# Attention tiles and feed-forward slices on one core: a longer tile pipeline, half weight loads, later stores, slices spread over all steps

## What is computed

```python
scores = scale * q @ k.T
kth = np.partition(scores, -32)[..., -32]
scores = np.where(scores >= kth, scores, -1e9)
x = softmax(scores) @ v
h = x @ w_in; x = (h * sigmoid(h)) @ w_out
P = exp(logits - max); 8 rounds of row and column scaling
out = sum over 8 experts of P[:, e] * (relu(x @ w1[e]) @ w2[e])
```

## Time and profile before

| what | value |
|---|---|
| median of three runs | 1378.49 us |
| the profiled execution | 1377.77 us |
| its span | 1376.0 us |
| mean granted TensorE clock | 0.968 |
| TensorE busy | 93% |
| VectorE busy | 50% |
| ScalarE, POOL busy | 30%, 27% |

### The profile page before, as it was taken

How to read it: one execution, slowest core, us unless ns; L and a number is a source line. 1 busy time by engine, 2 the same in 40 slices (tenths; PEclk the granted TensorE clock), 3 DMA queues, 4 the chain that set the end, 5 groups by cost and what they waited for, 6 DMA issues and landing times.

```text
span 1376.0 us, 21031 instructions
## 1 busy us (share of the span) xinstructions
PE 1284.8 (93%) x8029; PEld 1133.4 (82%) x8029; DVE 691.8 (50%) x1557; ACT 416.3 (30%) x888; POOL 365.4 (27%) x317
## 2 busy tenths in 40 slices
PE   5766699979979999999999999999999999999999
PEld 4555588768758889989989989989988988988997
DVE  6876899989999952652222222222222222222222
ACT  3433455445545523302202202202211211210210
POOL 2544433343434423202202202202202211211200
PEclk9987799989989999999999999999999999999999
DMA  4655514562543636211001001101101101101001
GB/s 122 210 201 188 197 71 172 192 210 88 229 158 138 246 129 245 73 51 61 32 31 62 30 30 61 42 19 61 61 0 61 61 0 61 61 22 39 0 0 69
DMA packets 72288, 130.12 MB, mean 95 GB/s; under 512 B 41376, under 2 KB 41376, under 8 KB 63008
## 3 DMA queue, kind: packets, MB, share of 16 engines
q1 hardware_dynamic: 72224, 129.27, 26.7%
HBM read 110.12 MB, written 19.14 MB: 94 GB/s over the span
## 4 chain that ended last, share of the span: by engine, by line
PE 75%; DVE 12%; POOL 6%; issue 3%; ACT 2%; DMA 2%; SPq 0%; ACTq 0%; DVEq 0%
PE banks L396 23%; PE banks L397 22%; PE banks L398 22%; DVE stats L838 5%; DVE rest L849 4%; PE banks L440 2%; POOL probs L1088 2%; DMA wu_raw<-in_moe_w_in_dram 2%; PE banks L464 1%; POOL wu_lo L1068 1%; PE banks L431 1%; DVE probs L860 1%; PE banks L549 1%; POOL wd_lo L1068 1%; POOL xt_lo L1094 1%
## 5 line engine op out<-in xcount | busy, mean ns | idle before, releaser
L798 ACT ACTIVATE h_hi<-banks 128x384 fp32r<-128x384 f32 x192 | 94.4, 492 | 624.6 <-PE banks L398 624.6
L396 PE MATMUL banks<-x_lo,wu_hi 128*128 128x384 f32 x768 | 257.2, 335 | 0.0
L398 PE MATMUL banks<-x_hi,wu_hi 128*128 128x384 f32 x768 | 256.8, 334 | 0.0
L397 PE MATMUL banks<-x_hi,wu_lo 128*128 128x384 f32 x768 | 256.8, 334 | 0.0
L1068 POOL TENSOR_TENSOR wu_lo<-wu_raw,wu_hi 128x512 fp32r<-128x512 f32 x76 | 95.9, 1300 | 580.7 <-ACT wu_hi L741 573.8
L969 DVE SCALAR_TENSOR_TENSOR h_lo<-banks,h_hi 128x384 fp32r<-128x384 f32 x192 | 106.8, 557 | 281.4 <-ACT h_hi L798 281.4
L1011 DVE SCALAR_TENSOR_TENSOR y_acc<-banks,plan_e,y_acc 128x512 f32<-128x512 f32 x135 | 101.4, 751 | 272.3 <-PE banks L398 272.3
L396 PE MATMUL banks<-wd_lo,h_hi 128*128 128x512 f32 x576 | 227.9, 396 | 0.0
L398 PE MATMUL banks<-wd_hi,h_hi 128*128 128x512 f32 x576 | 227.8, 396 | 0.0
L397 PE MATMUL banks<-wd_hi,h_lo 128*128 128x512 f32 x576 | 227.8, 396 | 0.0
L838 DVE MAX8 stats<-rest 128x8 f32<-128x576 f32 x216 | 156.1, 750 | 0.1
(11 more groups left out here) (102 smaller groups left out, 1876.3 us busy)
## 6 DMA issues: line engine op xcount, KB each, us to landing
wu_raw<-in_moe_w_dram SPq DMA_DIRECT2D x16, 1024.0 KB, 5.0
wd_raw<-in_moe_w_dram SPq DMA_DIRECT2D x16, 1024.0 KB, 5.1
wu_hi<-kept_up_hi SPq DMA_DIRECT2D x14, 1024.0 KB, 5.6
wu_lo<-kept_up_lo SPq DMA_DIRECT2D x14, 1024.0 KB, 7.8
wd_hi<-kept_down_hi SPq DMA_DIRECT2D x14, 1024.0 KB, 5.6
wd_lo<-kept_down_lo SPq DMA_DIRECT2D x14, 1024.0 KB, 8.1
q_nat<-in_q_dram SPq DMA_DIRECT2D x64, 72.0 KB, 2.1
wu_raw<-in_moe_w_in_dram SPq DMA_DIRECT2D x4, 1024.0 KB, 10.1
```

What stands on the lines that cost most here:

```text
L396: pe.matmul(to, a_hi, b_lo, start=first, stop=False)
L397: pe.matmul(to, a_lo, b_hi, start=False, stop=False)
L398: return pe.matmul(to, a_hi, b_hi, start=False, stop=last)
L798: act.activation(h_hi[:, f, CH * c:CH * (c + 1)], ps_up[:, at % UBANKS, 0:CH], ACT.Relu).then_inc(h_hi_done, 1)
```

## The change

All engines' orders in the step loops move. The distance from the scores to the values grows: TensorE weighs tile step - 3 before it makes new scores and transposes tile step - 2 after the second slice, and ScalarE copies the transposed tile step - 3 at the start of its step. VectorE's scaling goes behind its last removal, and the scalings' counterparts (the split of a group's output) run one to three steps later. Slices run at `slice_at(step, ...)` from position 4 on, spread over 18 steps with four steps that have only one; the table `PLACES` says which. Weight loads are cut in halves of 0.5 MB, asked for one and two steps after the old split began. Units 2 and 3 of each stream are stored at steps 19 to 22 (`KEEPS`) instead of at once. Fetches are issued a step after the last slice that reads the slot. The gate products of the first 768 tokens move from step `ALL` + 2 to `ALL` + 8, the last splits by three steps, and POOL's part of the sums is cut in two on two steps. No operation's size changes besides that one and the loads.

```diff
+FIRST_SLICE = 4
+SECOND_ALONE = (2, 7, 11, 16)
+PLACES = [(i, second) for i in range(NT) for second in range(2) if second or i not in SECOND_ALONE]
-STEPS = range(ALL + NT + 3)
+STEPS = range(ALL + NT + 5)
-          13: ("up", 3), 15: ("down", 3), ALL + 14: ("up", 4), ALL + 18: ("down", 4)}
+          13: ("up", 3), 15: ("down", 3), ALL + 17: ("up", 4), ALL + 21: ("down", 4)}
+KEEPS = {19: ("up", 2), 20: ("down", 2), 21: ("up", 3), 22: ("down", 3)}
...
 SP:
+            def load_half(stream, n, source, half):
+                parts = slice(half * PARTS // 2, (half + 1) * PARTS // 2)
+                need(sp, lo_split[stream], PARTS * (n - 1) + PARTS // 2 * (half + 1))
+                sp.dma_start(raw[stream][:, parts, :], source[:, parts, :]).then_inc(loaded[stream][half], 16)
-                begun = split_at(step - 3)
-                if begun:
-                    stream, n = begun
-                    if n < UQ:
-                        keep_unit(stream, n)
-                    load_split(stream, n + 1)
+                if split_at(step - 1):
+                    stream, n = split_at(step - 1)
+                    load_split(stream, n + 1, 0)
+                if split_at(step - 2):
+                    stream, n = split_at(step - 2)
+                    load_split(stream, n + 1, 1)
+                    if n < SLOTS:
+                        keep_unit(stream, n)
+                if step in KEEPS:
+                    keep_unit(*KEEPS[step])
...
 TensorE:
-                silu_slice(slice_at(step - 1, 0))
+                silu_slice(slice_at(step, 0))
+                if 0 <= step - 3 < ALL:
+                    weigh_values(step - 3)
                 if step + 1 < ALL:
                     scores_of(step + 1)
                 if 0 <= step - 3 < ALL:
                     spread_sums(step - 3)
-                if old:
-                    transpose_probs(step - 2)
-                if step == ALL + 2:
+                if step == ALL + 8:
...
-                silu_slice(slice_at(step - 1, 1))
+                silu_slice(slice_at(step, 1))
+                if 0 <= step - 2 < ALL:
+                    transpose_probs(step - 2)
                 transpose_head(head_at(step + 2), units_by(step - 3))
-                if old:
-                    weigh_values(step - 2)
...
 ScalarE:
+                if 0 <= step - 3 < ALL:
+                    copy_pT(step - 3)
+                g_high(slice_at(step - 1, 0))
+                if step % NT == 3 and NT <= step < ALL + NT:
+                    split_output(step // NT - 1, 2)
+                take_slice(slice_at(step, 0))
+                if 0 <= step - 2 < ALL:
+                    exp_scores(step - 2)
+                g_high(slice_at(step - 1, 1))
...
 VectorE:
-                if 0 <= step - 3 < ALL:
-                    scale_output(step - 3)
                 if new:
                     remove(step, 1)
-                take_slice(slice_at(step - 1, 0))
+                take_slice(slice_at(step, 0))
                 if 0 <= step - 2 < ALL:
                     guard_sum(step - 2)
+                if 0 <= step - 3 < ALL:
+                    scale_output(step - 3)
...
 POOL:
-                if step % NT == 3 and 2 * NT < step < ALL:
-                    sums_low(step // NT - 2)
+                if step % NT in (7, 8) and 2 * NT < step < ALL:
+                    sums_low(step // NT - 2, step % NT - 7)
```

More of the change, by code:

```diff
@@ L104, in slice_at, with step_of @@
 def slice_at(step, second):
-    quarter, p = step // NT - 1, 2 * (step % NT - 2) + second
-    return (quarter,) + SLICES[p] if quarter >= 0 and p >= 0 else None
+    quarter, place = (step - FIRST_SLICE) // NT - 1, ((step - FIRST_SLICE) % NT, second)
+    return (quarter,) + SLICES[PLACES.index(place)] if 0 <= quarter < QUARTERS and place in PLACES else None
+def step_of(stream, n, m):
+    return NT * (n // UQ + 1) + FIRST_SLICE + PLACES[SLICES.index((stream, n % UQ, m))][0]
 def split_at(step):
@@ L129, in fetches_at @@
 def fetches_at(step):
[L131 to L138, removed]
+    return [(stream, n) for stream in ("up", "down") for n in range(SLOTS, NU1)
+            if step_of(stream, n - SLOTS, UF - 1) + 1 == step]
 def slices_done(n, d):
@@ L271, in build @@
         logits_t_done, logits_copied = sem("logits_t_done"), sem("logits_copied")
-        loaded = {"up": sem("wu_loaded"), "down": sem("wd_loaded")}
+        loaded = {s: [sem("w_" + s + "_loaded" + str(i)) for i in range(2)] for s in ("up", "down")}
         hi_split = {"up": sem("wu_hi_split"), "down": sem("wd_hi_split")}
@@ L367, in _ @@
             load_head(0, 2)
-            load_split("up", 0)
-            load_split("down", 0)
+            for stream in ("up", "down"):
+                for half in range(2):
+                    load_split(stream, 0, half)
             for step in STEPS:
@@ L512, in silu_slice @@
                         pe.wait_ge(acc_set, KD * qr + m + 3)
+                    elif qr:
+                        pe.wait_ge(acc_added, KD * (qr - 1) + m + 3)
                     if m == 0:
@@ L556, in _ @@
             for step in STEPS:
-                old = 0 <= step - 2 < ALL
-                silu_slice(slice_at(step - 1, 0))
-                if step < NT:
+                silu_slice(slice_at(step, 0))
+                if step < NT + FIRST_SLICE:
                     keep_clock(ps_m[:, 1, 0:P], 4)
+                if 0 <= step - 3 < ALL:
+                    weigh_values(step - 3)
                 if step + 1 < ALL:
@@ L934, in _ @@
                     search(step, 0)
+                take_slice(slice_at(step - 1, 1))
                 if 0 <= step - 3 < ALL:
@@ L940, in _ @@
                     remove(step, 0)
-                take_slice(slice_at(step - 2, 1))
-                if step - 1 > ALL:
-                    split_pieces(pieces_at(step - 1, 1))
                 if old:
@@ L1099, in _ @@
                     lower_scores(step - 2)
-                g_low(slice_at(step - 2, 0))
-                g_low(slice_at(step - 2, 1))
+                if step % NT == 3 and NT <= step < ALL + NT:
+                    output_lows(step // NT - 1, 2)
+                g_low(slice_at(step - 1, 0))
+                g_low(slice_at(step - 1, 1))
                 if step < ALL:
```

67 lines of the change are left out of this document (29 added, 38 removed).

## The result

The changed kernel takes 1338.08 us as the median of four runs (1334.58 to 1341.57), the kernel before 1377.95 beside it. The ratio is 0.9708, 95% interval 0.9679 to 0.9737: 40 us faster. The profiled execution took 1338.02 us with a span of 1336.2.

What follows compares the result with a forecast made beforehand. It took the first quarter as bound by a 6.91 us tile loop through POOL, ScalarE and TensorE plus load waits, later quarters by VectorE with waits; 1377.77 - 28 - 12 + 2 = 1339.8, about 1340 us, range 1324 to 1360.

Steps and rivals of the forecast that it cites:

- ScalarE's copy a step later, and the loads: First quarter: POOL's loop shortens from 6.91 to 6.15 us a tile and load waits vanish; 28 us gained, ends 16 and 33.
- VectorE is the only limit: First quarter: the upper end, 33 us gained; with all stalls gone in every quarter, 1327 us, chance 0.05.
- the signs: What would show the forecast right, among them tile 17's compare near 127 us instead of 155.
- VectorE's own limit: First quarter: VectorE's work alone, 117 us plus 7 for compares that meet POOL, puts tile 17's compare at 124.
- Rival A: First quarter: other ScalarE work replaces the copy, so the period stays 6.9 us; whole 1353, chance 0.13.
- Rival D: First quarter: half loads issue no earlier, load waits stay and 13 of the 28 are lost; 1353, chance 0.05.
- Half loads, late stores: Weight loads and stores: cost zero; 3.5 us estimated for a half, two halves 7 instead of 5, hidden by distance.
- Slices and distances: Three later quarters: of 18 us in VectorE waits and long compares 6 stay, 12 gained, ends 4 and 18.
- Rival B: Later quarters: all 27 steps with POOL's second slice product lose 0.49 us at the compare; whole 1353, chance 0.10.
- The scaling at the end of the step: VectorE's step: waits for TensorE shrink, the next head's transposes wait for the scaling, thinly covered; zero.
- Rival C: Tile stage: head transposes wait for the moved scaling, 2 us in 32 head steps; 1404, chance 0.05 with its like.
- The tail: Behind the last compare: first slice after 12.1 instead of 14.2 us, gate products 4.2; net +2, ends 0 and +4.

Runs made afterwards that it cites:

- e1: The kernel before with only the change's loads and stores, every engine's order kept: 1364.32 us, ratio 0.990.
- e2: The changed kernel with the old times of loads and stores: 1356.58 us, ratio 0.984.
- e3: The changed kernel with ScalarE's copy of the transposed tile back in its old place: 1354.57 us, ratio 0.982.
- e6: The changed kernel with all units stored in the first quarter, right behind the second half load: 1336.55 us, ratio 0.9705.
- e10: The changed kernel with both load halves asked for together, two steps after the split began and ahead of the stores: 1335.80 us, ratio 0.969.
- e7: The changed kernel with every slice one step earlier: 1343.28 us, ratio 0.975.
- e4: The changed kernel with dense slices, two per step on the first 16 positions: 1335.87 us, ratio 0.970.
- e9: The changed kernel with POOL's part of the sums whole again: 1338.54 us, ratio 0.970.
- e5: The changed kernel with VectorE's scaling back ahead of its step's last removal: 1339.25 us, ratio 0.971.
- e11: The changed kernel run again, unaltered: 1340.44 us, ratio 0.9708.
- e8: The dense slices of e4 on the changed kernel, with 12 of the 24 gate products moved to step ALL + 2: 1332.66 us, ratio 0.9665.

## Why the prediction was right, and where it was not

The forecast was 1340, the median is 1338.08, and that the sum hit so closely is luck, two errors that cancel: 48.7 us were gained up to the last compare, where I had 40, and 8.7 lost behind it, where I had 2.

*ScalarE's copy a step later, and the loads: -28, measured -33.6*, just past the end of 33 that I gave to "VectorE is the only limit". The mechanism was right in both parts (e1, e2, e3), and so was the period of POOL's loop: 6.19 us in the mean, where I had 6.15. The failed pieces are the end of that sum and the 2 us taken off it. I let two tiles at VectorE's 5.6 (11.2 us) follow POOL's last lowering behind pieces, as if VectorE kept a fixed distance to POOL. It had drawn ahead, and compare 17 began only 121.78 - 114.86 = 6.9 us behind the lowering of tile 15: at 121.78, where the sum had 125.3 and the signs 127. VectorE's own limit was the better sum: 20.95 for the end of the first compare, 17 x 5.6 = 95.2 and 6.7 for blocked compares, 122.9; I had 124 and didn't use it. The two limits did not take turns so that both cost; POOL simply fell behind. Rival A (the loop keeps its length) is what e3 built, 122.7 us, and the change avoided it. Rival D fell: no weight-load waits.

*Half loads, late stores: zero, and so it is* (e6, e10). The Trainium skill, DMA: Bandwidth & Descriptors, section Rules for kernel authors, asks for at least 1 MiB per DMA where the most bandwidth is wanted. My estimate was 3.5 us for a half; in the experts, with nothing ahead, it landed after 3.7, and the experts, whose loads went from 1 MB to two halves, are the same to 0.2 us. I had written that the change touches no expert code, which these loads contradict. e10 shows that the early first half doesn't reach the time either.

*Slices and distances: -12, measured -15.1.* I had put 12 of waits and 5.7 of long compares together and kept 6. The waits fell from 12 to 1.1. The compares hardly improved: 55 x 0.608 - 55 x 0.51 = 5.4 us are still lost, of 5.7. Of the named causes only the distance of a step is shown, about 10 of the 15 (e7); the spreading and the cut sums, which I had listed as reasons too, showed no effect (e4, e9). Rival B (each compare with a POOL product loses 0.49) did not come: the mean stayed at 0.61. My reading of the long compare was a little off: it ends 0.31 us behind POOL's 2.64, not half a microsecond.

*The scaling at the end of the step: zero*, as e5 shows from the other side. Rival C, the head transposes that wait for it, was real as a wait (TensorE waits 3.4 us in two cases before key and query transposes and 1.9 in two more, in the whole trace); VectorE has no wait that comes from it.

*The tail: +2, measured +8.7; this term failed.* Its end was +4. Two pieces were wrong. First, the path: I let TensorE wait for the last tile's exponential (2.5 us) and counted three slices in the sum, though the text had five. TensorE waited for nothing there. Six slices, and the transposes and values of the tile before, were still ahead of it; the last tile's exponential ended at 451.13, and TensorE reached its transposes at 454.62, 7.2 us behind the compare (3.4 before the change). This put the first slice 17.1 us behind the compare, not 12.1, and 3.0 later than before, not 2.1 earlier. Only 1.5 of it is the fall of the clock (e9, e10). Second, behind the first slice 57.15 became 62.90: 4.2 for the gate products as reckoned, and 1.5 that I had not seen, of which 0.7 is TensorE's wait for a slice product queued on VectorE behind the split of the sums, 0.75 and 1.85 us, now in the middle of the slices. The remaining 0.8 I did not trace.

## What to carry to other kernels

When the tile stage belongs to one engine, look for a loop that leaves it: here a copy that stood between two stages on ScalarE closed a ring of 6.9 us round a 5.5 us engine, and moving that one copy gave as much as removing all load waits. Put a load ahead of the stores of its unit, far enough ahead of its use; asking for half of it earlier or thinning other traffic can then be left out. When two loops are almost equally long, ask which engine has to keep a distance to which: here VectorE could draw 4 us ahead of POOL, and its own sum gave the time. Work that slips behind the last item of the busy engine is paid there, so fill the gap with products that depend on nothing late, and count where the follower stands, not where the leader does.

## What the runs showed of the hardware

A compare that begins while more than 0.2 us of a POOL instruction are left ends 0.31 to 0.32 us behind that instruction, whichever of POOL's subtractions it is: all 23 compares over 0.6 us of the changed kernel's tile stage do, and the 2.81 us one before the change. It takes 0.51 alone.

The compare and POOL lock in one of two patterns, and the same kernel shows both. In the changed kernel's profile two weight pieces of 2.73 us together begin on POOL at 37.85, 0.31 us ahead of the compare, which takes 1.29: it begins while the first piece runs.

```profile
38.16 1.29 DVE L875 TENSOR_SCALAR probs<-scores,stats 128x576 f32<-128x576 f32 x1
```

In e11 the same two pieces, 2.52 us together, begin 1.31 us ahead of the compare, so that it begins when the second one has just started. POOL's rows:

```profile
38.36 2.52 POOL L1080 TENSOR_TENSOR wd_lo<-wd_raw,wd_hi 128x512 fp32r<-128x512 f32 x2 [2.19 <-ACT wd_hi L754]
41.27 1.41 POOL L1102 TENSOR_TENSOR probs<-scores,probs 128x576 f32<-128x576 f32 x1 [0.40 <-DVE probs L875]
```

and its compare of tile 3 on VectorE:

```profile
39.67 1.52 DVE L875 TENSOR_SCALAR probs<-scores,stats 128x576 f32<-128x576 f32 x1
```

POOL then waits 0.40 us for the compare. From tile 2 to tile 8 a tile takes a mean 6.16 us in one pattern and 6.39 in the other, with identical code, and that makes the 2.4 us of the first quarter. The Trainium skill, SBUF — State Buffer, section Who interferes with whom, under Practical consequences, says that when a VectorE instruction in a two-port mode meets a GpSimd one, whoever issues first keeps the shared pair for its whole instruction and the other blocks; the ends of the compares in both patterns and e9's 1.44 us agree with it, though no run tells the mode of the compare. A difference of 2 to 3 us in this kernel's first quarter is therefore no evidence for an edit, which is why e5 and e8 are not read there.
